# Local attention on merged 64-column scores: half the transposes, p.v on quarters of the array

## The reference: what is computed

```python
# q, k, v: (4, 8, 576, 64) fp32
pos = np.arange(S); rel = pos[:, None] - pos[None, :]
mask = (rel >= 0) & (rel < 64)                 # each row sees itself and 63 before it
scores = np.where(mask, scale * q @ k^T, -1e9)
attn = softmax(scores)                         # divided by (sum + 1e-9)
x = (attn @ v) laid out as (2304 tokens, 512)
x = relu(x @ w_in1)**2 @ w_out1                # 512 -> 2048 -> 512
h = x @ w_in2;  out = (h * cos(h)) @ w_out2    # 512 -> 2048 -> 512
```

## Time and profile before

| | before |
|---|---|
| median of 3 runs | 878.47 us (877.53 to 878.82) |
| profiled execution | 877.21 us |
| its span, first to last instruction | 875.4 us |
| PE busy | 859.8 us (98%) |
| DVE, ACT, POOL busy | 483.1, 376.9, 14.0 us |
| granted TensorE clock, whole run | 1.00 |

### The profile page before, as it was taken

The page is one execution under the profiler, slowest core; times in us unless marked ns, Lnnn a source line. Parts: engine busy times, 40 slices in busy tenths (PEclk is TensorE's granted clock), DMA queues, the critical chain, the costliest instruction groups (busy, mean ns, idle before and its releaser), DMA issues.

```text
span 875.4 us, 12810 instructions
## 1 busy us (share of the span) xinstructions
PE 859.8 (98%) x5064; PEld 739.5 (84%) x5064; DVE 483.1 (55%) x848; ACT 376.9 (43%) x833; POOL 14.0 (2%) x25
## 2 busy tenths in 40 slices
PE   6899999999999999999999999999999999999998
PEld 5799988888888888888999888899999888888886
DVE  6767554444434364423555765666666665556555
ACT  6556453334443443423446433444444343334333
POOL 3200000000000000000000000000000000000000
PEclk9999999999999999999999999999999999999999
DMA  7555231111401040020331000200200200001001
GB/s 260 181 168 185 82 111 47 56 55 61 144 25 55 32 151 25 1 97 1 109 126 55 0 1 1 86 36 1 96 37 1 97 37 1 0 1 49 1 0 49
DMA packets 18923, 55.08 MB, mean 63 GB/s; under 512 B 2096, under 2 KB 2096, under 8 KB 17840
## 3 DMA queue, kind: packets, MB, share of 16 engines
q1 hardware_dynamic: 18864, 54.27, 17.9%
HBM read 43.78 MB, written 10.49 MB: 62 GB/s over the span
## 4 chain that ended last, share of the span: by engine, by line
PE 95%; DVE 3%; ACT 1%; DMA 0%; issue 0%; DVEq 0%; ACTq 0%
PE h L436 34%; PE y L478 23%; PE y L517 22%; PE turned L436 6%; PE scores L436 5%; PE scores L410 2%; PE scores L383 1%; PE turned L398 1%; PE scores L398 1%; DVE arena L744 1%; PE y L383 0%; DMA arena<-qk_duos 0%; DVE neg_max L728 0%; DVE arena L723 0%; DVE g_lo L780 0%
## 5 line engine op out<-in xcount | busy, mean ns | idle before, releaser
L772 DVE TENSOR_TENSOR act<-act 128x512 f32<-128x512 f32 (+1 forms) x80 | 51.1, 639 | 213.4 <-ACT g_hi L616 213.4
L780 DVE TENSOR_TENSOR g_lo<-act,g_hi 128x512 fp32r<-128x512 f32 (+1 forms) x160 | 102.2, 639 | 54.3 <-ACT g_hi L621 51.6
L478 PE MATMUL y<-g_hi,w_out_hi 128*128 128x512 f32 (+1 forms) x320 | 121.0, 378 | 1.0 <-DVE g_lo L780 1.0
L436 PE MATMUL h<-x_hi,w_in_hi 128*128 128x512 f32 (+3 forms) x488 | 120.8, 369 | 0.7 <-ACT x_hi L589 0.7
L610 ACT ACTIVATE act<-h 128x512 f32<-128x512 f32 (+1 forms) x80 | 44.3, 554 | 177.1 <-PE h L436 177.0
L436 PE MATMUL h<-x_hi,w_in_lo 128*128 128x512 f32 (+3 forms) x488 | 119.2, 366 | 0.0
L436 PE MATMUL h<-x_lo,w_in_hi 128*128 128x512 f32 (+3 forms) x488 | 118.8, 365 | 0.0
L478 PE MATMUL y<-g_lo,w_out_hi 128*128 128x512 f32 (+1 forms) x320 | 117.9, 369 | 0.0
L478 PE MATMUL y<-g_hi,w_out_lo 128*128 128x512 f32 (+1 forms) x320 | 117.7, 368 | 0.0
L651 ACT ACTIVATE arena<-arena,half_pi 128x512 f32<-128x512 f32 (+1 forms) x80 | 54.5, 681 | 135.2 <-DVE arena L809 135.2
L517 PE MATMUL y<-w_out_hi,g_lo 128*128 128x512 f32 x288 | 112.7, 391 | 0.0
(11 more groups left out here) (98 smaller groups left out, 1036.8 us busy)
## 6 DMA issues: line engine op xcount, KB each, us to landing
arena<-qk_duos SPq DMA_DIRECT2D x17, 640.0 KB, 4.7
arena<-v_duos SPq DMA_DIRECT2D x18, 512.0 KB, 3.7
arena<-w_in SPq DMA_DIRECT2D x32, 256.0 KB, 2.7
arena<-w_out SPq DMA_DIRECT2D x32, 256.0 KB, 2.7
out<-arena SPq DMA_DIRECT2D x18, 256.0 KB, 2.1
x_tiles<-x_hi SPq DMA_DIRECT2D x2, 1024.0 KB, 4.0
x_tiles<-x_lo SPq DMA_DIRECT2D x2, 1024.0 KB, 6.9
x_hi<-x_tiles SPq DMA_DIRECT2D x2, 1024.0 KB, 5.0
```

Source lines behind the costliest of these rows:

```text
L436: mm = pe.matmul(to, w[:, f, k, :], x[:, k, :], start=(w is w_in_hi and x is hi and k == 0), stop=(x is lo and k == KC - 1))
L478: mm = pe.matmul(bank, w[:, f, d * P:(d + 1) * P], x[:, g % 2, c * size:(c + 1) * size], start=(s == 0 and c == 0 and n == 0 and d % per = ...
L772: nc.vector.tensor_tensor(a, a, a, ALU.mult).then_inc(sq_set, 1)
L780: nc.vector.tensor_tensor(g_lo[:, g % 2, cols], act[:, g % 2, cols], g_hi[:, g % 2, cols].bitcast(fp32), ALU.subtract).then_inc(glo_set, 1)
```

## The change

**Merged scores.** In a row i of a block the columns of the own block up to i count, and of the preceding block those beyond i. The two sets don't overlap, so the 128 columns are merged into 64: ACT copies the own block's scores out of PSUM (`own_scores`), and DVE puts the preceding block's scores over them where a mask says so (`merge_max`, with `copy_predicated`; in the first block of a sequence a constant takes their place). Row maximum, exponentials and norm then work on 64 columns for each pair. The scale goes onto q ahead of `qk`: by GpSimd for duos 1 to 17 (`scale_q`), by DVE and ACT for duo 0.

**Turning.** Two pairs (2 x 64 columns) are turned by one 128 x 128 transpose, so a block has two transposes and not four. DVE copies them out twice, each time multiplied by a triangle of ones (`spread`): once for the own block, once for the preceding one.

**p.v.** Keys of an even and an odd pair lie on the two halves of the partitions. A duo's p.v is 32 products, each 64 x 64 weights by 64 columns, in quarters of the array; own and preceding block are added up in PSUM. v is laid out on the host to fit and a duo loads 384 KB of it, not 512. PSUM banks are named in pairs.

**Order.** For the first four blocks the norm's product goes to GpSimd (`POOL_NORMS` is 4), which splits its second weight piece behind them. From duo 4 on, both blocks of a duo share one `merge_max` and one `norm`. On PE `turn(1)` goes ahead of `qk(2)`, `up_first(1, 0)` behind `pv(2)`, and the turning and p.v of duo 3 lie around `down1(1)`.

```diff
-    POOL_NORMS = 0
+    POOL_NORMS = 4
...
+                if d > 0:
+                    pe.wait_ge(qk_loaded[d % 2], 16 * (d // 2 + 1))
+                    pe.wait_ge(q_scaled, d)
...
+                for group in range(GROUPS):
+                    mm = pe.transpose(turn_bank(t)[:, group * P:(group + 1) * P],
+                                      prob_of(t)[:, 2 * group:2 * group + 2, :].rearrange("p a c -> p (a c)"),
+                                      ident[:, :])
...
+                    pe.wait_ge(prob_t_set, 2 * d + (b + 1 if d < FIRST_DUOS else 2))
+                    for group in range(GROUPS):
+                        for own in (True, False):
+                            for odd in range(2):
+                                for head in range(2):
+                                    rows, to = slice(odd * BLK, (odd + 1) * BLK), slice(head * HD, (head + 1) * HD)
+                                    cols = (group * 2 + (head ^ b)) * BLK
+                                    mm = pe.matmul(pv_cols(d)[to, odd, (group * 2 + b) * BLK:(group * 2 + b + 1) * BLK],
+                                                   v_at[d % 2][rows, b + own, group, head, :],
+                                                   prob_t[rows, b, 1 - own, cols:cols + BLK],
+                                                   start=own, stop=not own, tile_position=(odd * BLK, head * HD))
                 mm.then_inc(pv_done, 1)
...
             pe.wait_ge(ident_set, 1)
             turn(0)
+            turn(1)
             qk(2)
-            turn(1)
             pv(0)
             turn(2)
             turn(3)
             pv(1)
-            qk(3)
             turn(4)
             up_first(0, 0)
             turn(5)
+            qk(3)
+            pv(2)
             up_first(1, 0)
-            pv(2)
...
+                if g == 2:
+                    turn(2 * FIRST_DUOS)
+                    turn(2 * FIRST_DUOS + 1)
                 if g > 0:
                     down1(g - 1)
-                if d is not None and phase(j, s) == 2:
+                if g == 2:
+                    pv(FIRST_DUOS)
+                if d is not None and phase(j, s) == 2 and g > 1:
                     turn(2 * d)
                     turn(2 * d + 1)
...
+            def own_scores(t, count=1):
+                act_e.wait_ge(qk_done, t + count)
+                if t >= 4:
+                    act_e.wait_ge(turned, t + count - 4)
+                if t == 0:
+                    nc.scalar.mul(prob_of(t), scores_of(t)[1], SCALE).then_inc(own_set, 1)
+                else:
+                    nc.scalar.copy(prob_of(t, count), scores_of(t, count)[1]).then_inc(own_set, count)
...
+            own_scores(0)
+            own_scores(1)
             exps(0)
+            own_scores(2)
+            own_scores(3)
             exps(1)
             exps(2)
             exps(3)
-            copy_turned(0)
-            copy_turned(1)
+            own_scores(4)
+            own_scores(5)
+            x_high(0)
             exps(4)
-            copy_turned(2)
-            copy_turned(3)
-            x_high(0)
+            x_high(1)
             exps(5)
-            x_high(1)
-            copy_turned(4)
-            exps(6)
+            own_scores(6, 2)
             x_high(2)
-            exps(7)
...
+                        own_scores(2 * d, 2)
+                    if phase(j, s) == 1:
                         exps(2 * d)
-                    if phase(j, s) == 1 and g > 0:
                         exps(2 * d + 1)
-                    if phase(j, s) == 2:
-                        copy_turned(2 * d)
-                        copy_turned(2 * d + 1)
...
-            def mask_max(t):
-                of = prob_of(t)
-                dve.wait_ge(qk_done, t + 1)
-                if t // 2 >= FIRST_DUOS:
-                    dve.wait_ge(turned, t - 1)
-                elif t // 2 >= 2:
-                    dve.wait_ge(turned, t - 3)
-                entry = FIRST if t % SEQ_BLOCKS == 0 else GENERAL
-                nc.vector.scalar_tensor_tensor(
-                    out=of, in0=score_bank(t)[:, :].rearrange("p (a c) -> p a c", a=PAIRS),
-                    scalar=SCALE, in1=masks[:, entry:entry + 1, :].broadcast_to([P, PAIRS, WIN]),
-                    op0=ALU.mult, op1=ALU.add).then_inc(masked, 1)
-                dve.wait_ge(masked, t + 1)
...
+            def scale_second():
+                dve.wait_ge(second_loaded, 16)
+                nc.vector.tensor_scalar(q_cols(0)[:, 1, :], q_cols(0)[:, 1, :], SCALE, None, ALU.mult)\
+                  .then_inc(q_scaled_first, 1)
+            def merge_max(t, count=1):
+                dve.wait_ge(own_set, t + count)
+                first = [n for n in range(t, t + count) if n % SEQ_BLOCKS == 0]
+                for n in range(t, t + count, 1 if first else count):
+                    many = 1 if first else count
+                    mask = ahead[:, :].rearrange("p (o c) -> p o c", o=1).broadcast_to([P, many * PAIRS, BLK])
+                    others = scores_of(n, many)[0]
+                    if n in first:
+                        others = masked_score[:, :].rearrange("p (o c) -> p o c", o=1).broadcast_to([P, PAIRS, BLK])
+                    nc.vector.copy_predicated(prob_of(n, many), mask.bitcast(i32), others).then_inc(masked, many)
+                dve.wait_ge(masked, t + count)
+                nc.vector.tensor_reduce(neg_max[:, t % 4:t % 4 + count, :].rearrange("p n a -> p (n a)"),
+                                        prob_of(t, count), AX.X, ALU.max, negate=True).then_inc(maxed, count)
+            def invert(t, count=1):
...
+            def norm(t, count=1):
+                inv = invert(t, count)
+                dve.wait_ge(inverted, t + count)
+                inv = inv.rearrange("p (a o) -> p a o", o=1).broadcast_to([P, count * PAIRS, BLK])
+                nc.vector.tensor_tensor(prob_of(t, count), prob_of(t, count), inv, ALU.mult).then_inc(normed, count)
+            def spread(t):
+                d, b = t // 2, t % 2
                 dve.wait_ge(turned, t + 1)
-                if t >= 2:
-                    dve.wait_ge(pv_done, t // 2)
-                nc.vector.tensor_copy(prob_t[:, t % 2], turn_bank(t)[:, :].rearrange("p (a c) -> p a c", a=PAIRS))\
-                  .then_inc(prob_t_set[t % 2], 1)
+                if d >= 1:
+                    dve.wait_ge(pv_done, d)
+                shape = [P, 2, 2 * GROUPS, BLK]
+                columns = turn_bank(t)[:, 0:MERGED].rearrange("p (o n c) -> p o n c", o=1, c=BLK)
+                nc.vector.tensor_tensor(prob_t[:, b].rearrange("p w (n c) -> p w n c", c=BLK),
+                                        columns.broadcast_to(shape),
+                                        keep_t[:, :, :].rearrange("p w (o c) -> p w o c", o=1).broadcast_to(shape),
+                                        ALU.mult).then_inc(prob_t_set, 1)
...
-            dve.wait_ge(masks_set, 1)
-            mask_max(0)
-            mask_max(1)
-            mask_max(2)
-            norm(0)
-            mask_max(3)
-            norm(1)
-            mask_max(4)
-            norm(2)
-            norm(3)
-            mask_max(5)
+            nc.vector.memset(masked_score[:, :], MASKED).then_inc(consts_set, 1)
+            dve.wait_ge(consts_set, 4)
+            scale_second()
+            dve.wait_ge(masks_set, 3)
+            merge_max(0)
+            merge_max(1)
+            merge_max(2)
+            invert(0)
+            merge_max(3)
+            invert(1)
+            dve.wait_ge(masks_set, 8)
+            spread(0)
+            invert(2)
+            spread(1)
+            merge_max(4)
+            invert(3)
+            merge_max(5)
+            spread(2)
             x_low(0)
+            spread(3)
             norm(4)
             x_low(1)
+            spread(4)
             norm(5)
-            mask_max(6)
-            copy_turned(5)
-            mask_max(7)
+            spread(5)
+            merge_max(6, 2)
             x_low(2)
             for g in range(G1):
                 j, s, _ = steps1[g]
                 d = duo_in(j, s)
-                if d is not None and phase(j, s) == 2:
-                    norm(2 * d + 1)
+                if g == 2:
+                    spread(2 * FIRST_DUOS)
+                    spread(2 * FIRST_DUOS + 1)
...
-                        mask_max(2 * d + 1)
+                        merge_max(2 * d, 2)
                     if phase(j, s) == 1:
-                        norm(2 * d)
+                        norm(2 * d, 2)
+                    if phase(j, s) == 2 and g > 1:
+                        spread(2 * d)
+                        spread(2 * d + 1)
                     if phase(j, s) == 3:
...
+            def scale_q(d):
+                pool.wait_ge(qk_loaded[d % 2], 16 * (d // 2 + 1))
+                nc.gpsimd.tensor_scalar(q_cols(d), q_cols(d), SCALE, None, ALU.mult).then_inc(q_scaled, 1)
...
+            scale_q(1)
             w_split(0)
```

(31 more changed lines are left out.)

150 lines of the change are left out of this document (69 added, 81 removed).

## The result

| | before | after |
|---|---|---|
| median | 878.47 us (877.53 to 878.82, 5 runs) | 873.46 us (872.92 to 874.25, 5 runs) |
| profiled execution | 877.21 us | 873.09 us |
| its span | 875.4 us | 871.0 us |

The ratio of after to before is 0.9948, with a 95% interval of 0.9936 to 0.9959: faster by 5.0 us, or 0.5%. The forecast was 871 and 866 to 878.

A forecast was written before the change was run, and what follows sets the result against it. PE, busy 98% of the span, was taken to bound the kernel. Terms -6.1 - 2.3 + 1.0 = -7.4 on a profiled 877.2 gave 869.8; with the median 1.3 higher, 871 us, range 866 to 878.

The forecast's parts named there:

- Transposes, -6.1: PE's list, duos 4 to 17: four of eight transposes go, 0.43 us for each of 14 duos, 6.1 us saved.
- p.v at no cost: Each duo's p.v: 64 quarter products, four at once every 0.058 us, take 0.93 us again, as 32 records did.
- The serial rival: p.v quarter products go out one at a time: 64 records take 1.75 us, 14.7 us more, 886; chance 0.14.
- floor of the Trainium skill: Some 25 ns per short product; as serial floor 1.6 us per p.v instead of 0.93, 12 us in all, 883.
- Waits for `spread` in the first tile, +1.0: Duos 4 to 6: PE charged 0.3 us each waiting for spread, 1.0 in all, ends 0 and 1.5.
- The charge for duo 3: First tile: pv(3)'s two spreads queue on VectorE behind four weight splits, ending at 39.6; a new wait of 1.0 us.
- `scale_q(d)` of the later duos, norm and `spread` in the big tiles, nothing: 512-token tiles: scaling waits only for a load issued a duo's round earlier, norm and spread are covered; no cost.
- The front, -2.3: First 43 us, followed by latencies: up1(3) starts at 40.7 against 43.03, 2.3 us gained, ends 0 and 4.
- its first bullet: Start of the front: duo 1 lands at 6.1, is scaled until 6.9 (0.61 us), its scores last until 9.3.
- the front gains nothing: Rival for the first 43 us: scale_q costs 1.27, or similar; 873.4, or 875 with a 1.5 loss; chance 0.13.

The follow-up runs named there:

- turns_only: The kernel before with two transposes instead of four per block in duos 4 to 17, the other half of the turned scores left unset: 872.34 us, ratio 0.9932.
- own_inner: The changed kernel with p.v products reordered, own and preceding block innermost, so two successive products stay in one quarter: 877.22 us, ratio 0.9982 to before.
- spread_early: The changed kernel with VectorE doing duo 3's two spreads ahead of the second pair of weight splits: 871.63 us, ratio 0.9932 to before.
- norms_dve: The changed kernel with the norm products of the first four blocks on VectorE instead of GpSimd: 873.95 us, ratio 0.9967 to before.
- scale_dve: The changed kernel with q of duos 1 to 3 scaled on VectorE instead of GpSimd: 871.2 us, ratio 0.9916 to before.
- scale1_dve: The changed kernel with only duo 1's q scaled on VectorE instead of GpSimd: 871.55 us, ratio 0.992 to before.
- before_again: The last experiment: the kernel before, unedited, profiled once more to see how duo 1's load lands; one execution, 878.5 us, span 876.7.
- after_again: The changed kernel, unedited, profiled once more to see how duo 1's load lands; one execution, 872.37 us, span 870.2.

## Why the prediction was right, and where it was off

- **Transposes, -6.1.** Right: 0.79 to 0.36 us for a duo in the trace, 6.25 us by turns_only. One reading in it is off: "the next four as much", but 124.84 to 125.20 is 0.36 and not 0.43. It did no harm because the four that stay take 0.36 too, and so 0.43 goes; half of the 0.79 would have made 5.5.
- **p.v at no cost.** Right: 64 records in 1.09 us, 0.01 longer than the 32 were. The serial rival asked for 1.75 and is out. (So is the floor of the Trainium skill that the prediction cites, from TensorE: Matmul & The Clock Gate, "Back-to-back issue gap", as a serial cost: it makes an estimated 1.6 us, and the trace disagrees with 17 ns for each record.) own_inner adds what the prediction didn't know: that the price holds for this order of the quarters, and an order that stays in a quarter for two products pays 0.14 us a duo.
- **Waits for `spread` in the first tile, +1.0.** They didn't come: nothing on PE waits there behind 44 us. The charge for duo 3 (pv(3) "a new wait of 1.0") did come, as 0.91, at the place named, and spread_early removes it.
- **`scale_q(d)` of the later duos, norm and `spread` in the big tiles, nothing.** Right: 5.8 us of the 6.1 arrive.
- **The front, -2.3. This is the step that failed**, at its first bullet: "`scale_q` has no row; ... it lies between 0.61 and 1.27 and I take 0.61", and "Duo 1 lands at 1.6 + 4.5 = 6.1". The scaling is 1.49, outside both ends: one operand doesn't make it cheaper than two. The load took 6.5 in that execution. `qk(1)` came at 9.88 and not 6.9: 2.0 us of it the load, 0.9 the scaling. Then the chain is carried on with small changes: `turn(0)` 2.3 late; `turn(1)` 3.0, since the second scaling adds its 0.9 between the norms; `turn(4)` 3.6, with VectorE's norm of block 4 at 1.20 us beside a working GpSimd (the same form took 0.42 to 0.43 in norms_dve while GpSimd stood idle); `up1(3)` 3.7. With a scaling of 0.42 us, on VectorE, scale_dve and scale1_dve gain 1.9 to 2.3 us by their medians, so about that much hung on the price. The load's 2.0 belong to the execution and not to the change: before has them as well. By the medians of both kernels the front lost an estimated 0.5 us (last experiment) instead of gaining 2.3; the scaling accounts for 1.9 to 2.3 of these 2.8, and the rest stays open.

The sum by the profiled executions: -6.1 + 1.0 became -5.8, -2.3 became +1.4, so -7.4 became -4.4 in the span (875.4 to 871.0). That the forecast lies only 2.5 us from the median is in part luck: the front was forecast with the wrong sign, and the charge of 1.0 for waits that didn't come made up for some of it. The measured median is near the rival that "the front gains nothing", which was given 873.4 for just this cause (`scale_q` too dear), with 0.13. The range held because that rival was in it.

## What to carry to other kernels

What leaves a list that an engine works through without a pause can be counted well (0.43 us for each duo forecast and measured, 5.8 of 6.1 us in all); what moves in a start-up that lives on latencies can't, and should be given a range of its own and be checked by a second profile. An operation with no row is not bounded by rows of other operations on the same engine: a scaling of 512 columns took GpSimd 1.49 us and VectorE 0.42. Before work goes onto an idle engine, follow who waits for it: GpSimd was idle for 98% of the time, and still its 1.49 us stood on the path twice.

## What the runs showed of the hardware

- **GpSimd** takes 1.49 us to multiply 128 x 512 fp32 by a constant (L961 of the changed kernel), 1.26 for a two-operand step and 0.61 for a cast of that size; VectorE took 0.42 to 0.83 for the same multiplication in scale_dve.
- **Quarter products** of 64 x 64 by 64 columns start every 17 ns in a row when the quarters take turns (64 in 1.09 us), every 19 ns when two products in a row use the same quarter (64 in 1.23 us, own_inner).
- **A load's time isn't a constant**: 640 KB issued at 1.6 us landed after 4.5 in one execution of before and 6.3 in another; over all the profiled executions it was 4.5, 4.9, 5.3 and eleven times 6.1 to 6.5. What decides stays open.
- **TensorE's early pace**: the second score block took 1.98 us for 32 records at before_again's 8.03 and 1.10 at scale_dve's 7.93, and the granted clock in the rows falls to 0.5 for stretches of the first 40 us in 9 of 14 profiled executions; of the changed kernel's two, after_again has it from 10 to 20 us and after has none, though after's score products at 9.88 and 17.32 ran 1.99 long at a recorded clock of 1.00. So in the first 20 us the starts of the products tell more than the clock's row does.
